# Inverse blocks of a delta-rule attention worked on by two engines: three of the six rounds move from VectorE to GpSimd

## What is computed

```python
for t in range(S):                       # S = 768, batch 4, 8 heads, head size 48
    kt, vt, bt = (k_n[:, :, t], v[:, :, t], beta[:, :, t, None])
    y[:, :, t] = np.einsum('bhd,bhde->bhe', q[:, :, t], state)
    v_old = np.einsum('bhde,bhd->bhe', state, kt)
    state = state + bt[:, :, :, None] * np.einsum('bhd,bhe->bhde', kt, vt - v_old)
```

## Time and profile before

| | us |
|---|---|
| median of three runs | 1172.73 |
| lowest and highest run | 1171.76, 1173.15 |
| the profiled execution | 1171.63 |
| its span, first to last instruction | 1169.7 |
| steps n = 2 to 26 of the attention loop | 152.13 |

### The profile page before, as it was taken

One profiled execution on the slowest core, in us unless ns is written; L12 is line 12 of the kernel. 1 busy time (PEld: TensorE's weight loads), 2 busy tenths in 40 slices (PEclk: granted clock), 3 DMA queues, 4 the chain that ended last, 5 costly groups with the idle time before them and its releaser, 6 DMA issues.

```text
span 1169.7 us, 18004 instructions
## 1 busy us (share of the span) xinstructions
PE 1087.0 (93%) x6288; PEld 944.2 (81%) x6288; DVE 756.8 (65%) x1449; ACT 646.4 (55%) x1282; POOL 331.5 (28%) x313
## 2 busy tenths in 40 slices
PE   3349999999998899999999999999999999999998
PEld 3338899999997778888888888778888888888886
DVE  2767898888635998878888887876343333434332
ACT  3224666654447977777787877755333333333332
POOL 4000000000002887777777777710000000000000
PEclk9757999999999899999999999999999999999999
DMA  7957676854554201010010103033010101010000
GB/s 145 171 105 149 140 158 122 173 109 91 102 129 122 82 1 55 1 46 10 0 55 0 55 1 109 0 118 100 0 55 1 55 1 54 1 54 2 1 28 27
DMA packets 184250, 76.76 MB, mean 66 GB/s; under 512 B 146529, under 2 KB 172257, under 8 KB 183009
## 3 DMA queue, kind: packets, MB, share of 16 engines
q1 hardware_dynamic: 184160, 75.62, 27.4%
HBM read 53.58 MB, written 22.02 MB: 65 GB/s over the span
## 4 chain that ended last, share of the span: by engine, by line
PE 63%; DVE 4%; ACT 1%; issue 1%; ACTq 0%
PE ps_y L913 11%; PE ps_y L914 11%; PE ps_y L915 11%; PE ps_h L898 11%; PE ps_h L899 10%; PE ps_h L900 10%; DVE w_out_lo L1035 1%; DVE g_hi L1062 1%; DVE cubic L1047 1%; DVE w_in_lo L1032 0%; DVE g_lo L1077 0%; DVE ps_h L1069 0%; DVE ps_h L1053 0%; ACT w_in_hi L936 0%; DVE x_lo L1041 0%
## 5 line engine op out<-in xcount | busy, mean ns | idle before, releaser
L898 PE MATMUL ps_h<-x_hi,w_in_lo 128*128 128x512 f32 x576 | 226.0, 392 | 12.7 <-DVE g_lo L1077 5.9
L899 PE MATMUL ps_h<-x_lo,w_in_hi 128*128 128x512 f32 x576 | 225.5, 392 | 0.0
L900 PE MATMUL ps_h<-x_hi,w_in_hi 128*128 128x512 f32 x576 | 225.3, 391 | 0.0
L913 PE MATMUL ps_y<-g_hi,w_out_lo 128*128 128x512 f32 x576 | 224.4, 390 | 0.1
L914 PE MATMUL ps_y<-g_lo,w_out_hi 128*128 128x512 f32 x576 | 224.3, 389 | 0.0
L915 PE MATMUL ps_y<-g_hi,w_out_hi 128*128 128x512 f32 x576 | 224.1, 389 | 0.0
L1141 POOL TENSOR_SCALAR den_part<-h_sq,b_abs 128x512 f32<-128x512 f32 x96 | 72.1, 752 | 422.0 <-ACT h_sq L950 422.0
L1088 DVE TENSOR_TENSOR q<-h_sq 128x512 f32<-128x512 f32 x96 | 66.3, 691 | 135.7 <-ACT h_sq L977 134.1
L898 PEld LDWEIGHTS ps_h<-x_hi,w_in_lo 128*128 128x128 f32 x576 | 108.8, 189 | 37.2 <-issue 7.3
L984 ACT ACTIVATE g_hi<-q 128x512 fp32r<-128x512 f32 x96 | 60.7, 633 | 140.8 <-PE ps_y L915 136.2
L900 PEld LDWEIGHTS ps_h<-x_hi,w_in_hi 128*128 128x128 f32 x576 | 109.0, 189 | 22.8
(11 more groups left out here) (82 smaller groups left out, 1831.3 us busy)
## 6 DMA issues: line engine op xcount, KB each, us to landing
kq<-kq_in SPq DMA_DIRECT2D x12, 768.0 KB, 6.9
shared<-w_in SPq DMA_DIRECT2D x32, 192.0 KB, 4.3
shared<-w_out SPq DMA_DIRECT2D x32, 192.0 KB, 4.8
vkp<-k_in SPq DMA_DIRECT2D x12, 384.0 KB, 5.1
vkp<-v_in SPq DMA_DIRECT2D x12, 384.0 KB, 6.5
iq<-kq_in SPq DMA_DIRECT2D x12, 384.0 KB, 4.4
x_first<-y_t SPq DMA_DIRECT2D x24, 192.0 KB, 2.3
shared<-x_first SPq DMA_DIRECT2D x6, 768.0 KB, 5.9
```

The lines of the kernel that those rows point to most:

```text
L898: pe.matmul(bank(n), lo, x_hi[:, slot, k, :], start=(k == 0), stop=False)
L899: pe.matmul(bank(n), hi, x_lo[:, slot, k, :], start=False, stop=False)
L900: mm = pe.matmul(bank(n), hi, x_hi[:, slot, k, :], start=False, stop=(k == KT - 1))
L913: pe.matmul(ps_y[m][:, :], lo, g_hi[:, d, :], start=(f == 0), stop=False)
```

## The change

Rounds 1, 3 and 5 of the inverse are done by GpSimd, whole and one after the other, behind its constants; each waits only for its blocks. Rounds 0, 2 and 4 stay on VectorE; round 0 ahead of the loop as before, round 2 spread over the nine iterations n = 4 to 12 and round 4 over n = 20 to 28 (before: seven and eight, from 6 and from 21). Each engine has its own prod and its own step semaphore, each round its own inv_ready. The times at which SyncE asks for the inverse (INV_TO) and all its other places stay.

```diff
     INV_RING = 3
-    INV_FROM = (None, 0, 6, 13, 21, 29)
+    BY_POOL = (1, 3, 5)
+    INV_FROM = {2: 4, 4: 20}
     INV_TO = (None, 6, 13, 21, 29, 37)
-    INV_EARLY = 0
...
-        prod = sb("prod", [P, BL * BL // 4])
+        prod = [sb(f"prod{i}", [P, BL * BL // 4]) for i in range(2)]
...
             def store_inverse(r):
-                sp.wait_ge(inv_ready, r + 1)
+                sp.wait_ge(inv_ready[r], 1)
...
         @block.gpsimd
         def _(pool):
+            def invert(r, first, last):
+
+                x = inv[:, r % INV_RING]
+                for i in range(first, last):
+                    j, done = i // 2, (INV_OPS - 1) * (r // 2) + i
+                    if i == 0:
+                        pool.wait_ge(blk_loaded, 16 * r + 16)
+                        pool.tensor_tensor(x, x, upper[:, :, :], ALU.mult).then_inc(pool_inv_step, 1)
+                        continue
+                    pool.wait_ge(pool_inv_step, done)
...
+                        pool.tensor_tensor(part, x[:, 0:j, j:j + 1].to_broadcast(shape),
+                                          x[:, j:j + 1, j + 1:BL].to_broadcast(shape), ALU.mult
+                                          ).then_inc(pool_inv_step, 1)
+                    else:
+                        rest = x[:, 0:j, j + 1:BL]
+                        step = pool.tensor_tensor(rest, rest, part, ALU.add)
+                        step.then_inc(inv_ready[r] if i == INV_OPS - 1 else pool_inv_step, 1)
...
+            pool.wait_ge(const_ready, CONSTS)
+            for r in BY_POOL:
+                invert(r, 0, INV_OPS)
...
             def inverted(r, n):
 
-                early = INV_EARLY if r == 1 else 0
-                share = (INV_OPS - early) * (n - INV_FROM[r]) // (INV_TO[r] - INV_FROM[r])
-                return min(max(early + share, early), INV_OPS)
+                return INV_OPS * (n - INV_FROM[r]) // (INV_TO[r] - INV_FROM[r])
...
-            invert(1, 0, INV_EARLY)
             for n in range(LAST_MM):
-                for r in range(1, ROUNDS):
+                for r in INV_FROM:
```

More of the change, by code:

```diff
@@ L112, in build_attention @@
         blk_loaded = sem("blk_loaded")
-        inv_step = sem("inv_step")
-        inv_ready = sem("inv_ready")
+        dve_inv_step = sem("dve_inv_step")
+        pool_inv_step = sem("pool_inv_step")
+        inv_ready = [sem(f"inv_ready{i}") for i in range(ROUNDS)]
         inv_stored = sem("inv_stored")
@@ L295, in _ @@
         def _(pool):
+            def invert(r, first, last):
[7 more added lines that the diff above has]
+                    pool.wait_ge(pool_inv_step, done)
+                    part = prod[1][:, 0:max(j, 1) * (BL - 1 - j)].rearrange("p (c i) -> p c i", c=max(j, 1))
+                    if i == 1:
+                        diag = x.rearrange("p a b -> p (a b)")[:, 0:BL * BL:BL + 1]
+                        pool.tensor_tensor(diag, diag, upper[:, 0, 1:2].to_broadcast([P, BL]),
+                                          ALU.subtract).then_inc(pool_inv_step, 1)
+                    elif i % 2 == 0:
+                        shape = [P, j, BL - 1 - j]
+                        pool.tensor_tensor(part, x[:, 0:j, j:j + 1].to_broadcast(shape),
[5 more added lines that the diff above has]
+                        step.then_inc(inv_ready[r] if i == INV_OPS - 1 else pool_inv_step, 1)
             pool.memset(before[:, :], 1.0).then_inc(const_ready, 1)
@@ L619, in invert @@
                 for i in range(first, last):
-                    j, done = i // 2, (INV_OPS - 1) * r + i
+                    j, done = i // 2, (INV_OPS - 1) * (r // 2) + i
                     if i == 0:
                         dve.wait_ge(blk_loaded, 16 * r + 16)
-                        dve.tensor_tensor(x, x, upper[:, :, :], ALU.mult).then_inc(inv_step, 1)
+                        dve.tensor_tensor(x, x, upper[:, :, :], ALU.mult).then_inc(dve_inv_step, 1)
                         continue
-                    dve.wait_ge(inv_step, done)
-                    part = prod[:, 0:max(j, 1) * (BL - 1 - j)].rearrange("p (c i) -> p c i", c=max(j, 1))
+                    dve.wait_ge(dve_inv_step, done)
+                    part = prod[0][:, 0:max(j, 1) * (BL - 1 - j)].rearrange("p (c i) -> p c i", c=max(j, 1))
                     if i == 1:
@@ L629, in invert @@
                         dve.tensor_tensor(diag, diag, upper[:, 0, 1:2].to_broadcast([P, BL]),
-                                          ALU.subtract).then_inc(inv_step, 1)
+                                          ALU.subtract).then_inc(dve_inv_step, 1)
                     elif i % 2 == 0:
@@ L633, in invert @@
                         dve.tensor_tensor(part, x[:, 0:j, j:j + 1].to_broadcast(shape),
-                                          x[:, j:j + 1, j + 1:BL].to_broadcast(shape), ALU.mult).then_inc(inv_step, 1)
+                                          x[:, j:j + 1, j + 1:BL].to_broadcast(shape), ALU.mult
+                                          ).then_inc(dve_inv_step, 1)
                     else:
@@ L637, in invert @@
                         step = dve.tensor_tensor(rest, rest, part, ALU.add)
-                        step.then_inc(inv_ready if i == INV_OPS - 1 else inv_step, 1)
+                        step.then_inc(inv_ready[r] if i == INV_OPS - 1 else dve_inv_step, 1)
             def effective_q(n):
```

## The result

| | before | after |
|---|---|---|
| median | 1172.34 us (1171.76 to 1173.15, 4 runs) | 1180.11 us (1176.13 to 1182.63, 4 runs) |
| profiled execution | 1171.63 | 1176.13 |
| its span | 1169.7 | 1174.4 |

The changed kernel takes 1.0063 of the time before (95% interval 1.0034 to 1.0092): slower by 0.6%. Beside the last experiments it was measured once more on another chip: 1180.11 (1177.51 to 1183.50, 6 runs), ratio 1.0064 (1.0041 to 1.0086). The forecast was 1180.6. The total was right; several terms of its sum were not, and made up for each other. The experiments show which. Both profiled executions of the changed kernel were among the fast ones (1176.13, the fastest of 4, and 1178.96, the second fastest of 6), so what the profiles show is up to 4 us less than the medians.

The account below looks back on a forecast made before the run. TensorE, busy 93% of the span, was taken as the bound, with 10.5 us to win in steps 2 to 26. Terms +6.0, +0.5, -1.5, -1.6, +4.7 and -0.2 gave +7.9, so 1180.6 us; range 1178 to 1184.

Parts of the forecast that it names:

- steps 2 to 7 against before: Loop steps 2 to 7: step 8 starts 6.0 us later, the 0.8 won in steps 2 and 3 included.
- step 8: Step 8: ScalarE waits 1.6 us for k(8) instead of 1.08, +0.5.
- steps 9, 10: Steps 9 and 10: fewer inverse instructions on VectorE in iterations 8 to 10, -1.5 us.
- steps 14 to 18: Steps 14, 17 and 18: VectorE's relief wins back 1.6 us of 2.3 stall.
- step 21: Step 21: round 4's first instruction waits for blocks at n = 20, delaying the cross product by 4.7 us.
- the wait for blocks at n = 4 and n = 20: VectorE's queue: first instruction of rounds 2 and 4 waits for just-issued loads, with mq, z_diag and vkp behind it.
- rounds 3 and 5 are free on GpSimd: GpSimd's later rounds: round 3 has 58 us for 43.5 and a load of 5; round 5 is free by about 1.
- the mutual waits: VectorE and GpSimd excluding each other at SBUF: 2.9 us in step 5, about 3.0 in step 6.
- Rival (c): TensorE's clock falls at the stalls of steps 5 and 21: 1.5 us more each, up to 1184; chance 0.10.
- GpSimd's round: One inverse round on GpSimd takes 42 us; round 1 is held up some 2.5 more by VectorE.
- rival (a): GpSimd slower, a round of 47 us: round 1 holds step 8, round 5 is 4.2 late, 1189.8; chance 0.20.
- (b): VectorE's relief comes through: blocks land before VectorE asks, GpSimd's round under 38 us, 1165; chance 0.13.

Follow-up runs that it names:

- late_start: The changed kernel with rounds 2 and 4 begun one iteration later on VectorE (n = 5 and 21 instead of 4 and 20): 1174.69 us.
- empty_pool: The changed kernel with GpSimd's rounds 1, 3 and 5 cut to mask and diagonal, their 60 products and sums left out: 1175.01 us.
- pool_last_four: The changed kernel with rounds 2, 3, 4 and 5 on GpSimd instead of 1, 3 and 5; VectorE keeps 0 and 1: 1173.72 us.
- early_load: The changed kernel with SyncE loading the blocks of rounds 2 and 4 one iteration earlier (n = 2 and 18): 1180.34 us.
- after_again: The changed kernel once more, unchanged, with more repetitions: 1180.11 us, ratio to before 1.0064.
- late_early_k: The changed kernel with rounds 2 and 4 from n = 5 and 21 and the keys k(h) loaded one iteration earlier: 1169.41 us.
- later_early_k: late_early_k with round 2 from n = 6 instead of 5, as in the kernel before; early keys kept: 1169.23 us.

## Why the prediction was right, and where it was not

By its own steps, with the first and the second profile of after:

| | forecast | first | second |
|---|---|---|---|
| blocks of round 2, behind step 2's start | 17.0 | 17.7 | 16.8 |
| mask to z_diag(4) | 5.9 | 4.2 | 3.7 |
| z_diag to cross | 2.74 | 2.74 | 2.73 |
| cross(5) behind its step's start, less 2.4 | 6.2 | 5.1 | 3.7 |
| step 6 longer than 5.79 by | 3.0 | 1.55 | 0.96 |
| steps 2 to 7 against before | +6.0 | +3.6 | +1.5 |
| step 8 | +0.5 | +2.1 | 0.0 |
| steps 9, 10 | -1.5 | -1.55 | -1.55 |
| steps 14 to 18 | -1.6 | -1.3 | -1.5 |
| step 21 | +4.7 | +6.6 | +7.4 |
| steps 2 to 26 | +7.9 | +9.5 | +5.4 |

**Right.** What bounds the steps, that most of VectorE's relief lies beside the path, the wait for blocks at n = 4 and n = 20 and its whole chain to the cross product (late_start takes both stalls away), the small gains in steps 9, 10 and 14 to 18 to a few tenths, and that rounds 3 and 5 are free on GpSimd. VectorE's products, sums, masks and diagonals fell from 127.3 to 67.2 by the sum of their durations, 60 of the forecast 63; the rest is what the remaining ones wait for GpSimd. The page's busy time, which counts overlap once, fell by 50.9.

**The term that failed: the mutual waits.** 2.9 in step 5 and 3.0 in step 6 were worked out as if every VectorE instruction waited for one of GpSimd's. In the rows above the mask takes 0.45 longer than in empty_pool and three of the five small ones 0.3 to 0.4 longer (0.48 where empty_pool has 0.22, 0.62 where it has 0.19, 0.50 where it has 0.22), while the other two take no longer. The one of 0.19 follows the one of 0.62 at once: one wait for GpSimd let two through. Three to four waits instead of six or seven, and a step 6 that lost 0.96 to 1.55 instead of 3.0, make the price 1.9 to 3.0, not 5.9. The rule cited from the Trainium skill ("SBUF — State Buffer", Who interferes with whom) holds as a mechanism, most plainly in the 2.32 of pool_last_four; what was wrong was the number of times that it strikes.

**The term that was missing: the clock.** Rival (c) was given 0.10 as a case of its own; it happens together with the forecast. In step 21 the cross product began 7.95 behind the step's start, 0.85 more than forecast (2.4 + 4.7), since the load of blocks left 3.1 behind the start of step 20 instead of 2.2, with a y store in front of it that took 4.7 to issue. The other 1.0 (2.2 in the second profile) is TensorE at half clock, 0.72 of full on average there. In step 5 of the first profile, at 0.85, it cost only some 0.2, since the half clock fell mostly on matmuls that had time. Before, with stands of 1.4 at most, the clock had stayed at full.

**GpSimd's round**: 39.0 instead of 42 + 2.5, since 240 elements take 0.61 to 0.70, not 0.73, and VectorE held it up noticeably only twice, by 0.6 and 0.9. Its end, 130.15, was as early as VectorE's before. So rival (a) fell, and the inverse of round 1 did not gate step 8 in this kernel.

**Step 8** was priced right in kind and wrongly in size, +0.5 for k(8) against +2.1 and 0. The forecast had ScalarE's wait for k(8) end 13.3 behind round 1, and that held (13.7 and 13.5). But in the first profile round 1 ended 6 us earlier than forecast and step 8 began 7 earlier, and in the second 4.6 and 3.9, so the wait was 3.18 and 1.08 instead of 1.6. Its price is whatever TensorE has won by then. This didn't matter much to the forecast and decides the rivals: (b), VectorE's relief coming through, was priced at 1165, with the wait for k(8) gone, which grew instead. With the waits for blocks gone it is 1174.7 (late_start), and 1169.4 with the keys moved too. Without the move of k(8), no way of relieving VectorE in steps 2 to 7 that was tried here had step 9 start earlier than 149.43, 0.9 later than before.

So the errors cancel, and that 1180.1 stands against 1180.6 is partly luck. In the second profile the mutual waits were 4.0 too much and step 21 2.7 too little; its steps 2 to 26 come to 2.5 less than forecast, and 2.1 outside them, which the forecast put at nothing, make up for that. In the first the mutual waits were 2.9 too much, and step 8, step 21 and the later blocks 4.2 too little; 4.8 less ahead of step 2, by the clock of steps 0 and 1, then brought it under the forecast. How the 7.8 us between the medians are made up in a median execution, no profile shows.

Open: why early_load's median is no better than after's when its profiled steps are; why empty_pool's median fell by more than its steps; and what tells a stand that is followed by half clock from one (3.01) that isn't.

## What to carry to other kernels

Work moved to an idle engine is free only if its consumer is late and its inputs are early. The instruction to look at is the first one that the relieved engine runs instead: here it asked for a load that had just been issued, with the whole recurrence queued behind it. After taking away one wait, read which load or store is late next in the order of the DMA queue. Its time may be set by another engine's work and not move with the gain; the same one-line move of a load was worth about 1, 3 and 5 us, depending on what had been won before it. Two engines that exclude each other at a memory are costed by the length of the longer instruction and by how often they meet; keep long ones (a mask of 1024 elements, 2.4 us) away from a chain of short ones.

## What the runs showed of the hardware

- GpSimd runs a chain of small dependent products and sums over 128 partitions at 0.23 to 0.27 us for 30 elements and 0.61 to 0.70 for 240, with 0.08 between an instruction and the next that waits for it. A round of 62 takes 38.0 to 40.1 us, on VectorE without anything else 23.4.
- A VectorE sum over SBUF tiles of 0.32 us took 2.32 beside a GpSimd instruction of 2.44. A norm instruction of 0.17 (128x16, one SBUF input) took 2.27 in after where it met the mask of round 3, at 173.8.
- Most of the stands of TensorE listed under after_again came with 3.4 or 6.8 us at 1.2 instead of 2.4 GHz. In step 21 that added 1.0 and 2.2 us, in step 8 of late_early_k and later_early_k 1.7 and 2.3, in step 5 of after's first profile 0.2.
- The MoE part, the same in all kernels, took 802.5 to 805.8 us from one profile to the next.
